# Moving subtractions between GpSimd and VectorE in a kernel of retention and two feed-forward layers

## The reference

```
state = gamma * state + k_t v_t^T          (gamma differs by head)
y_t   = q_t . state / sqrt(64)
x     = y as (3072 tokens, 512)
h     = x @ w_in (512x1024); e = exp(h - max h); solu = h * e / (sum e + 1e-9)
ln    = (solu - mean) / sqrt(var + 1e-6) * g_ln;   x = ln @ w_out (1024x512)
h     = x @ w_in2 (512x2048);  out = (h * cos h) @ w_out2 (2048x512)
```

## Time and profile before

| | us |
|---|---|
| median of three runs | 986.65 |
| profiled execution, its own time | 986.37 |
| its span, first to last instruction | 984.3 |
| TensorE busy | 938.8 (95%) |
| VectorE busy | 732.1 (74%) |
| ScalarE busy | 562.8 (57%) |
| GpSimd busy | 298.1 (30%) |
| mean granted TensorE clock | 0.995 |

### The profile page before, as it was taken

How to read it: one execution, slowest core, us unless ns; L and a number is a source line. 1 busy time by engine, 2 the same in 40 slices (tenths; PEclk the granted TensorE clock), 3 DMA queues, 4 the chain that set the end, 5 groups by cost and what they waited for, 6 DMA issues and landing times. The chain is left out here.

```text
span 984.3 us, 14623 instructions
## 1 busy us (share of the span) xinstructions
PE 938.8 (95%) x4992; PEld 829.0 (84%) x4992; DVE 732.1 (74%) x1037; ACT 562.8 (57%) x922; POOL 298.1 (30%) x277
## 2 busy tenths in 40 slices
PE   2799999999999999999799999999999999999998
PEld 2688888888888888887699998999988899899997
DVE  6989899988999899987555667666665756766554
ACT  4655556656656656645464566545565546555463
POOL 5455576566575675642002000020000200000000
PEclk9899999999999999999999999999999999999999
DMA  7433264443563453525596534654435534363401
GB/s 257 130 98 113 87 227 163 156 165 133 182 218 112 147 194 133 174 103 172 206 342 201 171 108 118 204 161 118 118 113 176 183 115 117 107 185 116 125 11 64
DMA packets 106519, 148.18 MB, mean 151 GB/s; under 512 B 7408, under 2 KB 77040, under 8 KB 106480
## 3 DMA queue, kind: packets, MB, share of 16 engines
q1 hardware_dynamic: 106480, 147.69, 46.3%
HBM read 112.01 MB, written 35.65 MB: 150 GB/s over the span
## 5 line engine op out<-in xcount | busy, mean ns | idle before, releaser
L307 PE MATMUL bank<-yc_h,ring 128*128 128x384 f32 x448 | 153.0, 342 | 9.8 <-ACT e L857 4.0
L309 PE MATMUL bank<-yc_l,ring 128*128 128x384 f32 x448 | 151.9, 339 | 0.0
L310 PE MATMUL bank<-yc_h,ring 128*128 128x384 f32 x448 | 151.6, 338 | 0.0
L1133 DVE SCALAR_TENSOR_TENSOR gg<-turns,c 128x768 f32<-128x768 int32 x64 | 64.2, 1003 | 105.5 <-ACT turns L801 105.2
L307 PEld LDWEIGHTS bank<-yc_h,ring 128*128 128x128 f32 x448 | 84.5, 189 | 22.4 <-issue 15.1
L807 ACT ACTIVATE gg<-gg 128x768 f32<-128x768 f32 x64 | 54.1, 846 | 80.7 <-DVE gg L1140 80.4
L801 ACT ACTIVATE turns<-c 128x768 int32<-128x768 f32 x64 | 54.2, 847 | 79.7 <-DVE c L1203 76.8
L309 PEld LDWEIGHTS bank<-yc_l,ring 128*128 128x128 f32 x448 | 84.7, 189 | 6.6
L307 PE MATMUL bank<-w1o_h,z_h 128*128 128x512 f32 x192 | 79.3, 413 | 6.6 <-DVE z_l L1102 6.6
L310 PEld LDWEIGHTS bank<-yc_h,ring 128*128 128x128 f32 x448 | 84.5, 189 | 0.0
L752 ACT ACTIVATE work<-bank,nmax 128x1024 f32<-128x1024 f32 x24 | 26.8, 1117 | 98.3 <-DVE nmax L1069 98.3
(11 more groups left out here) (122 smaller groups left out, 2503.0 us busy)
## 6 DMA issues: line engine op xcount, KB each, us to landing
ring<-w_split SPq DMA_DIRECT2D x224, 256.0 KB, 2.8
w_split<-w_out SPq DMA_DIRECT2D x16, 896.0 KB, 4.5
w2o_split<-wo_out SPq DMA_DIRECT2D x16, 512.0 KB, 3.9
w2o<-w2o_split SPq DMA_DIRECT2D x8, 1024.0 KB, 8.2
raw<-kT SPq DMA_DIRECT2D x24, 256.0 KB, 2.7
raw<-qT SPq DMA_DIRECT2D x24, 256.0 KB, 3.0
raw<-kn SPq DMA_DIRECT2D x24, 256.0 KB, 3.8
raw<-vn SPq DMA_DIRECT2D x24, 256.0 KB, 4.4
```

The source lines that it names most:

```text
L307: eng.matmul(dst, ah, bh, start=first and i == 0, stop=False, skip_group_check=read_between)
L309: eng.matmul(dst, ah, bl, start=False, stop=False, skip_group_check=read_between)
L310: m = eng.matmul(dst, al, bh, start=False, stop=last_one and i == n - 1, skip_group_check=read_between)
L1133: dve.scalar_tensor_tensor(gg[:, r, :], turns[:, r, :], -TWO_PI_HI, flat(c_32[:, r, :, :]), ALU.mult, ALU.add)\
```

## The change

- While the pipeline fills (batch 0, tiles 0 and 1, `FIRST`), GpSimd only scales q and n; all low parts of k, q, v and n are subtracted on VectorE. GpSimd's low parts of the other tiles wait as well for the low part of the tile before.
- The SP queue loads the constants first, then k and q of tile 0. The loads of tile 1 and of the weight units alternate. GpSimd no longer waits for the zeroing of q_h and q_l.
- In period 1 the scores come first, and the splits of tile 1 are spread behind PL, DL and O0. The weight units 1 to 5 are split later.
- In the second half t_3, t_1 and t_2 of superblocks 1 to 3 are computed on VectorE, in rounds 4, 5 and 6 of the superblock before. The splits of the operands P6, P5 and P3 are done in round 7 in one group (the low parts behind `reduce2` of LO), P3 one slot group earlier than before.
- In every round c22 comes ahead of the LO `reduce` on VectorE. In the very first round c21 comes ahead of the LO sine on ScalarE.

```diff
@@ -60,6 +60,7 @@
 W1_UNITS = KD + K1 // 2
 W1_SLOTS = 4
 SETUP = 6
+FIRST = 2
 W2_UNITS = 2 * NJ
 PER_BATCH = 5
@@ -235,8 +236,8 @@
-        early = {(1, "PL"): (0,), (1, "O0"): (1,), (1, "PN"): (2,), (1, "O1"): (3,),
-                 (2, "PK"): (4,), (2, "PV"): (5,), (2, "CEN"): (6, 7)}
+        early = {(1, "PL"): (0,), (1, "PQ"): (1,), (1, "O1"): (2, 3),
+                 (2, "O0"): (4,), (2, "PN"): (5,), (2, "CEN"): (6, 7)}
         late = {(NT, "PL"): [("TA", 0)], (NT, "CEN"): [("YC", 0), ("YC", 1)],
                 (NT + 1, "T0"): [("YC", 2)], (NT + 1, "T1"): [("YC", 3)],
                 (NT + 1, "CEN"): [("YC", 4)]}
@@ -253,7 +254,7 @@
             if n == 0:
                 first = [("PK", 0), ("PQ", 0), ("PV", 0), ("PN", 0)]
             elif n == 1:
-                first = [("PK", 0), ("PV", 0), ("SC", 1), ("PL", 1), ("PQ", 0)]
+                first = [("SC", 1), ("PK", 0), ("PL", 1), ("DL", 1), ("O0", 1), ("PV", 0), ("PQ", 0)]
             elif n == 2:
                 first = [("PK", 0), ("PV", 0), ("SC", 1)]
             steps = first + [part for part in STEP if part not in first]
@@ -319,6 +320,10 @@
             return x.rearrange("p (h d) -> p h d", h=H)
+        def by_dve(t, b):
+
+            return isinstance(b, int) and b == 0 and t < FIRST
+
         def loaded(eng, loads, t, b):
             eng.wait_ge(loads[t % 2], b * (32 * TILES // 2) + 32 * (t // 2 + 1))
@@ -385,17 +390,25 @@
                     :, :, bass.ds(t * C, C)], yt32.rearrange("p (k t) -> p k t", k=KD))\
                     .then_inc(y_stored, 16)
-            for i, src in ((1, kT), (0, qT)):
-                sp.dma_start(raw[:, 0, i, :], src[0, :, :]).then_inc(ld_kq[0], 16)
+            def load_kq(t, par):
+                for i, src in ((1, kT), (0, qT)):
+                    sp.dma_start(raw[:, par, i, :], src[t, :, :]).then_inc(ld_kq[par], 16)
+
+            def load_nv(t, par):
+                for i, src in ((2, kn), (3, vn)):
+                    sp.dma_start(raw[:, par, i, :], src[t, :, :]).then_inc(ld_nv[par], 16)
+
             sp.dma_start(cst[:, 0:MASK0], consts[:, 0:MASK0]).then_inc(ld_cst, 16)
-            for i, src in ((2, kn), (3, vn)):
-                sp.dma_start(raw[:, 0, i, :], src[0, :, :]).then_inc(ld_nv[0], 16)
+            load_kq(0, 0)
+            load_nv(0, 0)
             sp.dma_start(cst[:, MASK0:NCONST], consts[:, MASK0:NCONST]).then_inc(ld_mask, 16)
             sp.dma_start(g_col[:, :], g_ln).then_inc(ld_mask, 16)
             load_w1(0)
-            load_tile(1, 1)
-            for u in range(1, W1_SLOTS):
-                load_w1(u)
+            load_kq(1, 1)
+            load_w1(1)
+            load_nv(1, 1)
+            load_w1(2)
+            load_w1(3)
             load_next(0, 0)
             for u in range(W1_SLOTS, W1_UNITS):
                 load_w1(u)
@@ -874,16 +887,19 @@
                     turn(i, j, LO)
                     if j == NJ - 1 and more:
                         y_hi(i + 1, P5)
+                        y_hi(i + 1, P3)
                 else:
-                    sine(i, j, LO)
+                    begin = first and j == 0
+                    if not begin:
+                        sine(i, j, LO)
                     at(act, p_done[P4], i, j)
-                    if j > 0 or not first:
+                    if not begin:
                         at(act, g_done[HI], i, j - 1)
                     act.copy(c_32[:, HI, 0, :], ps_x).then_inc(c21_done, 1)
+                    if begin:
+                        sine(i, j, LO)
                     turn(i, j, HI)
                     square(i, j, LO)
-                    if j == NJ - 1 and more:
-                        y_hi(i + 1, P3)
@@ -916,22 +932,30 @@
                     q = raw[:, par, 0, :]
                     loaded(pool, ld_kq, t, b)
                     pool.tensor_tensor(q, q, qsc, ALU.mult).then_inc(q_sc, 1)
+                    if by_dve(t, b):
+                        return
                     wait(pool, k_hi, b, t)
+                    wait(pool, k_lo, b, t - 1)
                     subtract(k_l[:, par, :], raw[:, par, 1, :], k_h[:, par, :]).then_inc(k_lo, 1)
                 elif name == "PV":
                     k = heads(raw[:, par, 2, :])
                     loaded(pool, ld_nv, t, b)
                     pool.tensor_tensor(k, k, ksc.unsqueeze(2).broadcast_to([128, H, D]),
                                        ALU.mult).then_inc(n_sc, 1)
+                    if by_dve(t, b):
+                        return
                     wait(pool, v_hi, b, t)
+                    wait(pool, v_lo, b, t - 1)
-                elif name == "PQ":
+                elif name == "PQ" and not by_dve(t, b):
                     wait(pool, q_hi, b, t)
+                    wait(pool, q_lo[0], b, t - 1)
-                elif name == "PN":
+                elif name == "PN" and not by_dve(t, b):
                     wait(pool, n_hi, b, t)
+                    wait(pool, n_lo, b, t - 1)
@@ -965,11 +989,8 @@
             def y_sums(i):
                 pool.wait_ge(ld_y, i * 16 + 16)
-                if isinstance(i, int) and i == 0:
-                    pool.wait_ge(q_lo[1], NT)
-                    pool.wait_ge(n_lo, NT)
-                else:
-                    block_wait(pool, yl_done, i, 7, P7 - 7)
+                pool.wait_ge(q_lo[1], NT)
+                pool.wait_ge(n_lo, NT)
                 combine(t_3, b22, b12, ALU.subtract).then_inc(t3_done, 1)
                 block_wait(pool, t3_done, i, 1, 0)
                 combine(t_1, b12, b11, ALU.subtract).then_inc(t1_done, 1)
@@ -983,10 +1004,8 @@
                 combine(t_4, b21, t_2, ALU.subtract).then_inc(t4_done, 1)
             pool.wait_ge(ld_cst, 16)
-            pool.wait_ge(setup, SETUP)
             run(pool, step)
             with pool.Fori(1, NS) as i:
-                y_sums(i)
                 y_sum4(i)
@@ -1004,8 +1023,27 @@
             def step(name, t, b):
                 par = t % 2
                 c = t % TILES
-                if name == "PQ":
+                if name == "PK" and by_dve(t, b):
+                    wait(dve, k_hi, b, t)
+                    dve.tensor_tensor(k_l[:, par, :], raw[:, par, 1, :],
+                                      k_h[:, par, :].bitcast(F32), ALU.subtract)\
+                        .then_inc(k_lo, 1)
...
+                elif name == "PQ":
                     wait(dve, q_hi, b, t)
+                    if by_dve(t, b):
+                        dve.tensor_tensor(q_l[0:64, par, :, 0, :], raw[0:64, par, 0, :].rearrange(
+                            "p (c t) -> p c t", c=PAIRS), q_h[0:64, par, :, 0, :].bitcast(F32),
+                            ALU.subtract).then_inc(q_lo[0], 1)
                     dve.tensor_tensor(q_l[64:128, par, :, 1, :], raw[64:128, par, 0, :].rearrange(
                         "p (c t) -> p c t", c=PAIRS), q_h[64:128, par, :, 1, :].bitcast(F32),
                         ALU.subtract).then_inc(q_lo[1], 1)
@@ -1127,6 +1165,18 @@
                 dve.tensor_tensor(yc_l[:, p, :, :], operand[p], yc_h[:, p, :, :].bitcast(F32),
                                   ALU.subtract).then_inc(yl_done, 1)
+            def y_sum(i, p):
+                if p == P7:
+                    dve.wait_ge(ld_y, i * 16 + 16)
+                    block_wait(dve, yl_done, i, 7, P7 - 7)
+                    dve.tensor_tensor(t_3, b22, b12, ALU.subtract).then_inc(t3_done, 1)
+                elif p == P5:
+                    block_wait(dve, t3_done, i, 1, 0)
+                    dve.tensor_tensor(t_1, b12, b11, ALU.subtract).then_inc(t1_done, 1)
+                else:
+                    block_wait(dve, t1_done, i, 1, 0)
+                    dve.tensor_tensor(t_2, b22, t_1, ALU.subtract).then_inc(t2_done, 1)
+
             def reduce(i, j, r):
                 at(dve, turn_done[r], i, j)
@@ -1179,8 +1229,6 @@
                     dve.tensor_tensor(c_32[:, LO, 0, :], ps_y2, e_1[:, :], ALU.add)\
                         .then_inc(c11_done, 1)
                     before(g_lo, i, j, LO, first)
-                    if j == 0 and not first:
-                        y_lo(i, P3)
                 elif p == P6:
                     before(gate, i, j, HI, first)
                 elif p == P5:
@@ -1191,6 +1239,8 @@
                         out_copy(i - 1, 1)
                     elif j == NJ - 1 and more:
                         y_lo(i + 1, P1)
+                    elif j > NJ - 5 and more:
+                        y_sum(i + 1, {NJ - 4: P7, NJ - 3: P5, NJ - 2: P6}[j])
                 elif p == P3:
                     if j == 0 and not first:
                         y_lo(i, P4)
@@ -1205,18 +1255,17 @@
                 elif p == P7:
                     if j == 1 and not first:
                         out_copy(i - 1, 5)
-                    reduce(i, j, LO)
                     at(dve, p_done[P7], i, j)
                     at(dve, e5_done, i, j)
                     dve.tensor_tensor(c_32[:, HI, 1, :], ps_x, e_5[:, :], ALU.add)\
```

(26 more changed lines are left out.)

## The result

The kernel after took 976.60 us (median of four runs, 976.22 to 977.44), the kernel before beside it 986.82 (984.34 to 988.37). The ratio is 0.990, 95% interval 0.988 to 0.992. The forecast was 977.0. The profiled execution took 976.69 us, 9.7 less than before's 986.37. In its page TensorE is busy for 937.3 us. The second line is the chain of waits that ended last; VectorE has 20% of it, and I come back to that at the end. (The page before follows its chain over only 13% of the span, so the two can't be compared.)

A forecast was written before the change was run, and what follows sets the result against it. TensorE, busy 938.8 of 984.3 us, was taken to set the pace, leaving only 45.5 us idle to win. Filling 5.5, first round 0.5, superblock starts and sums 3.4: 9.4 off 986.37 gives 977.0 us, range 972 to 983.5.

The forecast's parts named there:

- The filling: Pipeline start, tiles 0 and 1: inputs reach TensorE sooner, 5.5 us gained and kept from 57 us on.
- the two exchanged stalls: Tile 1: `p_m` and `p_l` move ahead of four w1o_l; 2.86 us idle vanish, O0 starts at 31.2 to 31.8.
- The wait of several us for `x_l` at 42: Filling, tile 1: the second `x_l`, behind two moved weight units, ends at 42.5 us instead of 48.05.
- GpSimd's four scalings: Filling, tiles 0 and 1: spaced by data arrival, they don't hold VectorE, so `k_l` ends at 15.1, `p_l` at 15.75.
- Rival (a): Filling: VectorE stands behind GpSimd at 25 and 37 us; filling gives only 2, total time 980.5 us; chance 0.13.
- The clock: Before the second `x_l`: TensorE idles, matmuls may start at 1.2 GHz, 2.3 us at most, included in the 5.5.
- The first round: Start of the second half: c22 and c21 come sooner, saving 0.5 us (0 to 2) of 6.2 idle.
- The starts of the superblocks and the sums: Second half: e_5 sooner at three starts, 2.5 us, and the stall at 777 us gone, 0.9: together 3.4 us.
- (b): The second `x_l` lands where it was; 0.5 remains of the filling, 2 of the second half: 984 us; chance 0.08.
- (c): More gain: no contention in the filling, 7.5, and the first round gives 2: 973.5 us; chance 0.09.
- (d): Second half: delayed LO sine holds c21 in 31 rounds; at 1.7 us delay the time is 992; chance 0.04.
- from 57 us on TensorE has no slack left: Behind the filling: TensorE has no slack, so it keeps the filling's gain of 5.5 us.

The follow-up runs named there:

- kernel 1: Against the kernel before, only the filling is changed (low parts of tiles 0 and 1 on VectorE, new order of loads and steps): 982.34 us, ratio 0.9957.
- kernel 11: The kernel after with only the last w1_out weight unit (7) moved to just behind PL of period 3: 976.21 us, ratio 0.9890 to the kernel before.
- kernel 10: The kernel after with one more GpSimd wait: v is scaled only once both p_l of the tile before are written: 962.56 us, ratio 0.9745 to before.
- 8: The kernel after with the first round's reordering undone (table load and first sine ahead of the c21 copy): 975.35 us, ratio 0.9881 to the kernel before.
- 3: Against the kernel before, only the low parts of tiles 0 and 1 moved to VectorE, old orders kept: 985.82 us, ratio 0.9992.
- kernel 4: Against the kernel before, only loads, steps and weight units in the new order, low parts still on GpSimd: 983.72 us, ratio 0.9968.
- kernel 12: The kernel before with only one more GpSimd wait: v is scaled only once both p_l of the tile before are written: 969.05 us, ratio 0.9826.
- 2: Against the kernel before, only the second half is changed (sums, operand splits, c22 and c21 orders), filling as before: 980.43 us, ratio 0.9945.
- 5: Against the kernel before, only the splits of the operands P6, P5 and P3 are moved: 980.81 us, ratio 0.9942.
- kernel 6: Against the kernel before, only c22 is moved ahead of the LO reduce: 982.37 us, ratio 0.9958.
- 7: Against the kernel before, only the sums t_3, t_1, t_2 of superblocks 1 to 3 are moved to VectorE: 985.45 us, ratio 0.9992.

## Why the prediction was right, and where not

The total, 977.0 against 976.6, is the sum of three terms of which each was off.

The filling was forecast at 5.5 and is worth 4.4 in the steady tiles, 3.3 from 216 us on (4.3 by the medians of kernel 1). The steps: the first matmul at 9.6 came at 10.19 here (its `q_l`, from 8.03, took 1.30 us beside GpSimd's scaling), at 9.53, 9.85 and 10.09 with the same filling in kernels 11, 10 and 8. O0 at 15.8 came at 16.60, O1 at 19.1 at 19.88. The step of the two exchanged stalls was right: no wait at O0 of tile 1, which came at about 32.8 (31.2 to 31.8). The wait of several us for `x_l` at 42 came as three, of 1.86, 1.04 and 1.36 us, and the second `x_l` ended at about 43.6 instead of 42.5.

The step that failed in this term is the sentence that GpSimd's four scalings don't hold VectorE. One of them, from 14.35 to 15.39, held `k_l`, which ended at 15.95 instead of 15.1, and `p_l` and O0 behind it are 0.8 us late. It shows best in kernel 11: its first matmul is 0.66 us sooner and `k_l` starts at 14.36, but takes 1.54 us beside the same scaling and ends at 15.90, and O0 comes at 16.56 all the same. From O0 of tile 1 to the end of the second `x_l` there passed 10.8 us, and about 11 were forecast, although `q_l` took 1.78 us there instead of 0.69, beside GpSimd's n_l (2.47 in the kernel before): that was within the price, and the last 1.1 us is the lateness from ahead of it.

Rival (a) took 3.5 us off the filling for the lock. It fell short by 1.1, and by 1.1 more at 216 us. I had looked for the gain first at the starved `p_l`; kernels 3 and 4 give most of it to the orders, and kernel 12 shows that freeing `p_l` with a wait on GpSimd gives the same 4 us at 48 us. Both together (kernel 10) give 4.9 there, so the two don't add.

The rule of the Trainium skill that I weighed (SBUF — State Buffer, Who interferes with whom) says that the engine which starts first holds the shared ports for its instruction and the other blocks. The traces of the new orders agree with it in size too: `k_l` above, `s_l` (1.79 us) and the two operations of the pair at 214.88 (1.59 and 1.77) or of the one in kernel 4 (1.46 and 1.77) each take longer than alone by about one GpSimd instruction or less. It fails where GpSimd works without a pause: the first `p_l` of 4.93 us, beside four instructions, comes again with 4.92 or 4.93 in kernels 2, 5, 6 and 7, which fill the pipeline as before, and in kernel 12 a w1i_l of 1.21 us took 4.28 (21.62 to 25.90) beside three. Where GpSimd pauses after one instruction, as in kernel 12 at 14.49, `p_l` takes 2.29. What decides between taking turns and standing still stays open.

The clock did as forecast: granted 0.50 to 0.55 from 40 to 48 us, and the slack before 57 us covered most of it: the gain went from 4.46 to 2.9 at the low clock and was 4.07 again at the 56.86 row.

The first round was forecast at 0.5 and gave 0.05 up to its last wait (486.56 before, 483.16 after); the low clock behind it is in both traces. Of the two edits c22 is worth 0.4 and c21 costs 0.3. c21 and the table load changed places as foreseen, but that e_1 stands behind them on ScalarE I had not counted.

The starts of the superblocks and the sums were forecast at 3.4 and gave 6.1. Here the mechanism was right (no wait for e_5, none at 777, none for c12) and the size wrong: the term priced a wait at its idle time. The starts, with 0.48 to 0.56 and 0.31 to 0.35 us of idle time, cost some 1.6 each (0.2 of it at a matmul 4 us ahead of e_5's, where the profile shows no idle time), and the one of 0.93 us cost 1.2.

The misses, -2.2, -0.5 and +2.7, cancel; that the total came within 0.4 us is luck. Rivals (b), (c) and (d) didn't come; of (d) one wait of 0.21 us is seen in kernel 6. What the prediction overlooked is not in the change: it says that from 57 us on TensorE has no slack left, and the steady tiles held 14 us.

## What to carry to other kernels

Price a wait of TensorE at its idle time plus some 0.25 us, and add up the small ones of the steady loop by group before looking at the large ones that occur once: 21 waits of 0.2 to 0.8 us were worth more here than the whole filling. Where VectorE and GpSimd both work in SBUF, let the engine with slack wait for the one on the path; one such wait gave 14 to 17 us, and moving the work between them about 1. Test the parts of a sum one by one even when the total fits. And follow the gain matmul by matmul: it parts an edit worth 0.3 us from a stretch of low clock worth 1.5, which the end of a single trace does not.

## What the runs showed of the hardware

VectorE with two SBUF inputs, started at the same moment as GpSimd in the trace (214.88 us), took 3.28 us for a pair that takes 1.28 alone (1.59 and 1.77 for its two operations); beside four GpSimd instructions without a pause one operation took 4.93 us in place of 0.69. With GpSimd held back, the median of the 42 `p_l` operations from 60 to 448 us fell from 1.53 to 0.68 us. A wait costs TensorE its idle time and about 0.25 us (0.80 for 0.56 at 597 us). After 2.24 us of idle time the granted clock was 1.2 GHz in one execution of the same piece of program (the kernel after) and 2.4 in another (kernel 11), worth about 1.5 us.
